# Output weight remainders on VectorE, three of them inside the experts' last step, and one input weight remainder on GpSimd

## What is computed

```
attn = softmax(q k^T / 8 - slope * distance, masked) v        # 2 x 8 heads, 768 tokens, 64 wide
x    = sum_e p[:, e] * (relu(attn @ w1[e]) @ w2[e])           # 1536 tokens, 512 -> 1024 -> 512, 4 experts
h    = x @ w_in                                               # 512 -> 1024
solu = h * softmax(h)
ln   = (solu - mean(solu)) / sqrt(var(solu) + 1e-6) * g_ln
out  = ln @ w_out                                             # 1024 -> 512
```

## Time and profile before

| | |
|---|---|
| time, median of 3 runs | 753.35 us |
| the profiled execution | 753.5 us, span 751.7 us |
| TensorE busy | 744.6 us, 99% of the span, 3994 passes |
| TensorE's weight loads busy | 652.9 us, 87% |
| VectorE busy | 525.5 us, 70% |
| ScalarE busy | 218.9 us, 29% |
| GpSimd busy | 341.0 us, 45% |
| granted TensorE clock | 1.000 |

### The profile page before, as it was taken

One profiled execution on the slowest core, in us unless ns is written; L12 is line 12 of the kernel. 1 busy time (PEld: TensorE's weight loads), 2 busy tenths in 40 slices (PEclk: granted clock), 3 DMA queues, 4 the chain that ended last, 5 costly groups with the idle time before them and its releaser, 6 DMA issues. The chain is left out here.

```text
span 751.7 us, 12616 instructions
## 1 busy us (share of the span) xinstructions
PE 744.6 (99%) x3994; PEld 652.9 (87%) x3994; DVE 525.5 (70%) x1042; ACT 218.9 (29%) x414; POOL 341.0 (45%) x326
## 2 busy tenths in 40 slices
PE   9999999999999999999999999999999999999998
PEld 8888899899898998989988898898898877888876
DVE  5677767676666766767666676676767799867772
ACT  5677641111111111111211112111113743433332
POOL 4367546253542535425354253543535974442400
PEclk9999999999999999999999999999999999999999
DMA  9756310100101000010000100000022100000001
GB/s 263 194 142 167 105 31 2 56 29 29 31 26 56 28 28 28 28 56 28 28 28 28 56 28 28 28 28 0 1 112 66 49 0 15 15 29 28 16 28 42
DMA packets 39106, 37.15 MB, mean 49 GB/s; under 512 B 14497, under 2 KB 31905, under 8 KB 39073
## 3 DMA queue, kind: packets, MB, share of 16 engines
q1 hardware_dynamic: 37472, 34.64, 15.0%
q10 hardware_dynamic: 1600, 2.10, 0.8%
HBM read 33.59 MB, written 3.15 MB: 49 GB/s over the span
## 5 line engine op out<-in xcount | busy, mean ns | idle before, releaser
L809 PE MATMUL y_ps<-w2s,hs 128*128 128x512 f32 x1140 | 286.0, 395 | 0.1
L789 PE MATMUL p_ps<-xs,ws 128*128 128x384 f32 x1344 | 255.2, 336 | 0.0
L809 PEld LDWEIGHTS y_ps<-w2s,hs 128*128 128x128 f32 x1140 | 212.4, 188 | 41.0 <-DVE acc L1474 0.6
L789 PEld LDWEIGHTS p_ps<-xs,ws 128*128 128x128 f32 x1344 | 237.6, 188 | 11.0
L1474 DVE SCALAR_TENSOR_TENSOR acc<-y_ps,pr,acc 128x512 f32<-128x512 f32 x178 | 133.0, 748 | 79.6 <-PE y_ps L809 78.6
L1121 ACT ACTIVATE hs<-hs_sum 128x384 fp32r<-128x384 f32 x128 | 67.4, 527 | 353.6 <-DVE hs_sum L1442 238.9
L1461 DVE SCALAR_TENSOR_TENSOR hs<-hs_sum,hs 128x384 fp32r<-128x384 f32 x128 | 93.2, 737 | 4.3 <-ACT hs L1121 2.2
L577 POOL TENSOR_TENSOR ws_sum<-raw_sum 128x256 f32<-128x256 f32 x16 | 11.8, 739 | 146.8 <-PE p_ps L789 146.0
L608 POOL CAST w2s<-raw_sum 128x1024 fp32r<-128x1024 f32 x16 | 16.9, 1056 | 86.1 <-PE y_ps L809 86.1
L1134 ACT ACTIVATE neg_s<-neg_s,row 128x256 f32<-128x256 f32 (+1 forms) x96 | 42.2, 483 | 26.0 <-DVE row L1493 25.9
L1493 DVE CUSTOM_DVE_ANT_0 neg_s<-s_ps,bias 128x256 f32<-128x256 f32 (+1 forms) x96 | 34.3, 399 | 20.2 <-PE s_ps L823 18.1
(11 more groups left out here) (152 smaller groups left out, 971.2 us busy)
## 6 DMA issues: line engine op xcount, KB each, us to landing
raw_sum<-in_w SPq DMA_DIRECT2D x28, 512.0 KB, 3.5
qk<-in_qkW SPq DMA_DIRECT2D x24, 256.0 KB, 3.7
qk<-in_qkW SPq DMA_DIRECT2D x24, 128.0 KB, 4.1
v_sb<-in_v SPq DMA_DIRECT2D x16, 192.0 KB, 3.0
out<-o_sb SPq DMA_DIRECT2D x12, 256.0 KB, 2.0
raw_sum<-in_w ACTq DMA_DIRECT2D x4, 512.0 KB, 7.0
raw_sum<-in_w_in SPq DMA_DIRECT2D x1, 2048.0 KB, 8.0
wout_lo_a_sum<-in_w_out SPq DMA_DIRECT2D x1, 1792.0 KB, 7.6
```

Source lines behind the costliest of these rows:

```text
L789: mm = nc.tensor.matmul(bank, ws[slot][:, w, part, kk, :], xs[:, 2 * bt + kk, x, part, :], start=(kk == 0 and w == 1 and x == 1), stop=(kk ...
L809: mm = nc.tensor.matmul(mixed_at(s, t), hs[bt][:, h, b, tok], w2s[slot][:, w, f, :], start=(f == 0 and h == 1 and w == 1), stop=(f == 1 an ...
```

## The change

ScalarE's scaling in place (L1264) is gone, and all eight chunks of `w_out` are scaled and rounded in one instruction. The remainders of all eight are made on VectorE by the operation that chunks 4 to 7 had. Those of chunks 0, 1 and 2 stand inside VectorE's list for step 31, those of 3 and 4 between the last four `add_up`, those of 5 to 7 where they were. The sixth input weight remainder goes from VectorE to GpSimd. VectorE's loop over the steps ends one round (four steps) earlier, and steps 28 to 31 are written out.

```diff
-    WIN_POOL = 5
+    WIN_POOL = 6
...
-            def split_wout(c):
-                pool.wait_ge(wouthi_ready, c + 1)
-                pool.sem_inc(pool_waited, 1)
-                nc.gpsimd.tensor_tensor(wout_lo(c), wout_raw(c), f32(wout_hi(c)), ALU.subtract).then_inc(wout_ready, 1)
...
             for q in range(2):
-                for c in range(2):
-                    split_wout(2 * q + c)
                 x2_sums(q)
                 x2_los(q)
...
                         if s == 0:
-                            pe.wait_ge(wout_ready, FC // 2)
-                            pe.wait_ge(wout_split, FC // 2)
+                            pe.wait_ge(wout_ready, FC)
...
             def wout_hi_part(c):
-                if c < FC // 2:
-                    act.wait_ge(wout_scaled, c + 1)
-                    nc.scalar.activation(wout_hi(c), wout_raw(c), ACT.Copy).then_inc(wouthi_ready, 1)
-                else:
-                    nc.scalar.activation(wout_hi(c), wout_raw(c), ACT.Copy, scale=gain_sb[:, c:c + 1]
-                                         ).then_inc(wouthi_ready, 1)
+                nc.scalar.activation(wout_hi(c), wout_raw(c), ACT.Copy, scale=gain_sb[:, c:c + 1]).then_inc(wouthi_ready, 1)
...
             for c in range(FC // 2):
-                scale_wout(c)
+                wout_hi_part(c)
             relu_hi(LAST, 3, 1)
-            for c in range(FC // 2):
-                wout_hi_part(c)
             relu_hi(LAST, 2, 1)
...
+            def wout_lo_part(c):
+
+                if c == 0:
+                    dve.wait_ge(gain_loaded, 16)
+                dve.wait_ge(wouthi_ready, c + 1)
+                nc.vector.scalar_tensor_tensor(wout_lo(c), wout_raw(c), gain_sb[:, c:c + 1], f32(wout_hi(c)),
+                                               ALU.mult, ALU.subtract).then_inc(wout_ready, 1)
+
             def halve(a, i):
...
                 third_sum(s, i)
+                if isinstance(a, int) and s == LAST:
+                    wout_lo_part(0)
                 add_up(s - 1, 3, 1 - bt, expert, first)
...
                 lower_block(s, i)
+                if isinstance(a, int) and s == LAST:
+                    wout_lo_part(1)
+                    wout_lo_part(2)
                 right_block(s, i)
...
-            with dve.Fori(1, STEPS // 4) as a:
+            with dve.Fori(1, STEPS // 4 - 1) as a:
                 for i in range(4):
                     halve(a, i)
+            for i in range(4):
+                halve(STEPS // 4 - 1, i)
...
             for t in range(4):
                 add_up(LAST, t, 1, E - 1)
-                if t in (0, 2):
-                    win_lo_part(WIN_POOL + t // 2)
+                if t == 1:
+                    win_lo_part(WIN_POOL)
+                    wout_lo_part(3)
+                if t == 3:
+                    wout_lo_part(4)
...
             def first_pair():
-                wout_lo_part(4)
                 wout_lo_part(5)
```

More of the change, by code:

```diff
@@ L360, in attention_experts_solu_kernel @@
         winlo_dve = sem("winlo_dve")
-        wout_scaled = sem("wout_scaled")
         wouthi_ready = sem("wouthi_ready")
         wout_ready = sem("wout_ready")
-        wout_split = sem("wout_split")
         p_done = sem("p_done")
@@ L1255, in wout_hi_part @@
             def wout_hi_part(c):
-                if c < FC // 2:
-                    act.wait_ge(wout_scaled, c + 1)
-                    nc.scalar.activation(wout_hi(c), wout_raw(c), ACT.Copy).then_inc(wouthi_ready, 1)
-                else:
-                    nc.scalar.activation(wout_hi(c), wout_raw(c), ACT.Copy, scale=gain_sb[:, c:c + 1]
-                                         ).then_inc(wouthi_ready, 1)
-            def scale_wout(c):
-                nc.scalar.activation(wout_raw(c), wout_raw(c), ACT.Copy, scale=gain_sb[:, c:c + 1]).then_inc(wout_scaled, 1)
+                nc.scalar.activation(wout_hi(c), wout_raw(c), ACT.Copy, scale=gain_sb[:, c:c + 1]).then_inc(wouthi_ready, 1)
             act.wait_ge(win_loaded, 16)
@@ L1662, in _, with win_lo_part @@
                 attend_wide()
+            def win_lo_part(at):
+                n = WIN_ORDER[at]
+                dve.wait_ge(winhi_ready, at + 1)
+                nc.vector.tensor_tensor(win_lo_at(n), win_sum_at(n), f32(win_hi[:, n]), ALU.subtract
+                                        ).then_inc(winlo_dve, 1)
+            def wout_lo_part(c):
[4 more added lines that the diff above has]
+                                               ALU.mult, ALU.subtract).then_inc(wout_ready, 1)
             def halve(a, i):
@@ L1688, in _ @@
                 halve(0, i)
-            with dve.Fori(1, STEPS // 4) as a:
+            with dve.Fori(1, STEPS // 4 - 1) as a:
                 for i in range(4):
                     halve(a, i)
-            def win_lo_part(at):
-                n = WIN_ORDER[at]
-                dve.wait_ge(winhi_ready, at + 1)
-                nc.vector.tensor_tensor(win_lo_at(n), win_sum_at(n), f32(win_hi[:, n]), ALU.subtract
-                                        ).then_inc(winlo_dve, 1)
-            def wout_lo_part(c):
-                if c == FC // 2:
-                    dve.wait_ge(gain_loaded, 16)
-                dve.wait_ge(wouthi_ready, c + 1)
-                nc.vector.scalar_tensor_tensor(wout_lo(c), wout_raw(c), gain_sb[:, c:c + 1], f32(wout_hi(c)),
-                                               ALU.mult, ALU.subtract).then_inc(wout_split, 1)
+            for i in range(4):
+                halve(STEPS // 4 - 1, i)
             for t in range(4):
                 add_up(LAST, t, 1, E - 1)
-                if t in (0, 2):
-                    win_lo_part(WIN_POOL + t // 2)
+                if t == 1:
[3 more added lines that the diff above has]
+                    wout_lo_part(4)
             def negated(q, n, m, half, other):
```

## The result

The changed kernel took 754.58 us at the median of 20 executions (753.84 to 755.53), the kernel before 753.41 (753.29 to 753.88, 20 executions). The ratio is 1.0015, interval 1.0009 to 1.0022: 1.2 us slower, a difference clear of zero but inside the 1.5 us that the prediction counts as no change. The forecast was 754.0, its range 752.5 to 755.6.

What follows compares the result with a forecast made beforehand. TensorE, 99% busy, was taken as the bound, with VectorE's chain second and setting the end after 616. TensorE's net +0.6 and VectorE's +0.8 gave some +0.7 us on 753.35: 754.05, stated as 754.0, range 752.5 to 755.6.

Steps and rivals of the forecast that it cites:

- Output remainder 0: VectorE, step 31: held by GpSimd's second input remainder, runs 589.3 to 590.0; `lower_block` 0.5 us late, nothing waits.
- Output remainders 1 and 2: VectorE ahead of `right_block`, step 31: GpSimd blocks them, `mix(31, 0)` starts about 598.0, TensorE loses 2.85 us.
- The rule of turns: Two-SBUF-input VectorE and SBUF-reading GpSimd instructions exclude each other; whoever began finishes, then the waiter goes; up to 2.5 us each.
- What comes back: TensorE up to the second pair's first `up`: waits of 0.19, 0.1, 0.3 and 1.67 us (for L742) vanish.
- the sum there: TensorE at the second pair's first `up`: 2.85 us lost less the returned waits leaves +0.6 us.
- VectorE's chain in the second pair: Tail: `largest(0)` waits out the second L742, `solu_part(0)` starts +0.8 us later, and that shift moves the end.
- At nothing: ScalarE's dropped roundings, the moved input remainder, remainders 3 and 4, steps written out: 0, code fetch bounds -0.2 and +1.
- Rival A: Step 31: blocking weaker than scheduled, `mix(31, 0)` only 0.1 us late, -2.2 us, 751.2; chance 0.09.
- Rival B: Ahead of `mix(31, 0)`: GpSimd gets two more turns of 0.74, TensorE loses 4.3, total +2.2, 755.6; chance 0.15.
- Rival C, the clock: New 2.85 us gap before `mix(31, 0)`: clock falls to 1.2 GHz, two slow `mix` add +2.8, 756.9; chance 0.05.

Runs made afterwards that it cites:

- e3_pool5: The changed kernel with the sixth input weight remainder back on VectorE, so GpSimd has five instead of six; 753.87 us, ratio 1.0005.
- e4_behind_relu: The changed kernel with output remainders 1 and 2 moved behind both `relu_lo` of step 31; 753.28 us, ratio 0.9996.
- e8: The repeated run: the changed kernel once more, without an edit; 754.39 us, ratio 1.0013 against the kernel before.
- e1_filled_gap: The changed kernel with nine unread matmuls in TensorE's gap ahead of `mix(31, 0)`; 754.01 us, ratio 1.0006.
- e5_pool_splits_late: The kernel before, with two of GpSimd's four output splits moved behind `spread(0)`, past the second `L742`; 753.45 us, ratio 1.0001.
- e9_pool_splits_gated: e6 with GpSimd's two splits held back until VectorE has done three small two-operand instructions (L1779 to L1781); 752.01 us, ratio 0.9983 against the kernel before.
- e10_mid_filled: e6 with six unread matmuls ahead of `up(1, 5)`, where TensorE waited 1.86 us; 753.12 us, ratio 0.9994 against the kernel before.
- e2_written_out: The kernel before, with only VectorE's last four steps written out instead of looped; 753.67 us, ratio 1.0002.
- e6: The kernel before, with two of GpSimd's four output splits moved directly behind the second pair's `L742`; 753.46 us, ratio 0.9998.
- e7: The changed kernel with output remainder 3 also ahead of `right_block` in step 31; 756.33 us, ratio 1.0038 against the kernel before.

## Why the prediction was right, and where it was not

The forecast schedule held nearly row by row, and at full clock it gave the number: 754.1 against 754.05 worked out on the median. Two parts of that are luck. The growth of the distance in the trace is 0.52, and 0.7 was forecast; the rest lies in when `mix(30, 5)` starts, which differs between executions (593.61 to 594.22 in the traces) and for which the prediction has no term. And the median stayed inside "no change" only because fewer than half of the executions had a fall of the clock: those that did are 2.0 us above the kernel before.

- *Output remainder 0.* Forecast to end at 590.0 behind GpSimd's second input remainder; it ended at 589.86 after 2.40 us. Right.
- *Output remainders 1 and 2.* Forecast to issue at 593.1 and end at 596.95; they issued at 592.97 and ended at 596.53. `mix(31, 0)` at 597.64 (forecast 598.0), a loss of 2.6 us for the 2.85 forecast. The rule of turns was right, and the turns came somewhat sooner than written: the sixth input remainder ended at 594.86 (595.0), the sum between the two remainders at 595.99 (596.3). `e3_pool5` showed that 1.8 of the loss came with the sixth input remainder, which the step names, and `e4_behind_relu` that it is the place ahead of `right_block` that exposes TensorE to it.
- *What comes back.* The wait for `L742` went. At full clock 2.53 us came back up to `up(1, 1)` (distance 20.56 before, 20.62 in the repeated run), where 2.26 were forecast: 0.27 at `up(0, 1)`, 0.08 at the next turn, 0.45 in the first pair, 1.76 at `L742`, against 0.02 more in `mix`. So the sum there was +0.06 and not +0.6. That term was mis-sized, by 0.26 in the loss and 0.27 in the return. Most of the second comes from a misread base: 0.44 us from `turn_x` to the next pass, taken as undisturbed, is not. A later pair of the same trace has 0.35, and the pairs of the changed kernel have 0.35 or 0.36:

```profile
617.15 0.60 PE L950 MATMUL xr_ps<-ident,acc 128*128 128x128 f32 x4
617.50 0.48 PE L1028 MATMUL up_ps<-win_hi,x 128*128 128x512 f32 x1
```

- *VectorE's chain in the second pair.* It saved the number, since it and not TensorE's list sets the end. `largest(0)` issued at 613.81 and was held to 615.79 (forecast 614.0 and 615.9); `solu_part(0)` came 0.54 to 0.67 later, forecast 0.8; the distance to the end grew by 0.52. The 0.5 us that TensorE had regained went into its next wait for `stats`, 0.74 in place of 0.25. The traces without a fall of the clock show which chain sets the end. Change of distance against the kernel before, us:

| | `up(1, 1)` | `solu_part(0)` | `up(1, 5)` | end |
|---|---|---|---|---|
| changed (`e8`) | +0.06 | +0.54 | +0.55 | +0.52 |
| `e1_filled_gap` | +0.09 | +0.57 | +0.59 | +0.63 |
| `e3_pool5` | +0.48 | +0.37 | +0.39 | +0.37 |
| `e4_behind_relu` | -0.67 | -0.19 | -0.16 | -0.15 |
| `e5_pool_splits_late` | -2.14 | -1.53 | -1.51 | +0.04 |
| `e9_pool_splits_gated` | -2.18 | -1.57 | -1.55 | -1.48 |
| `e10_mid_filled` | -2.15 | -1.54 | -0.47 | -0.46 |

The end does not follow `up(1, 1)`. It follows `solu_part(0)`, but for `e10`, where that instruction itself is held up for 1.1 us by the splits, and `e5`, where VectorE's chain is held up behind it.

- *At nothing.* The steps written out cost nothing that shows (`e2_written_out`).
- *Rival A* fell with the first remainder's 2.40 us. *Rival B* did not occur, no further turn was lost. Its price was added up wrongly: 2.85 and two turns of 0.74 make 4.33, less the return of 2.26 some +2.1, which is 755.4 and not 755.6; the upper end of the range hangs on it.
- *Rival C, the clock.* This is what the prediction had wrong. It got a chance of 0.05, because nothing in the trace showed a fall. It happened in 8 of 20 executions and in 3 of 11 of the repeated run. Its price was also mis-sized: not two `mix` at half speed (+2.8), but 3.4 us of them, 1.52 us at TensorE and 1.35 at the end (755.45 to 754.1). The first four passes ran at full clock before the fall. With this share the median of 20 comes to 754.58 rather than 754.1. `e1_filled_gap` and `e10_mid_filled` point to TensorE's idleness as the cause: the same delays with TensorE busy, and no fall in 22 executions, with the chips as the one rival left.

The Trainium skill's warning ("TensorE: Matmul & The Clock Gate", section "Why this matters for your kernels") that a gap can bring the lower clock back was cited in the prediction as something no run showed. Here the runs show it, at idle times of 2.4 and 1.9 us. The row of that section is about longer gaps than these, so here the measurement decides.

What stays open: why only a part of the executions fall. TensorE's longest idle time near the place was 1.5 us in the kernel before (none of the 80 executions with a clock on record below 0.999), 1.9 in `e6` (7 of 11), 2.4 in the changed kernel (11 of 31), 3.6 in `e7` (4 of 5). With so few executions neither an even growth with the idle time nor its absence is shown. No run moved one gap in time alone, and no filled kernel is on record beside its unfilled one on the same chip.

## What to carry to other kernels

Price a VectorE instruction with two SBUF operands by what GpSimd does in that moment, and schedule both engines as taking turns: remainders of one form were 0.74 or 2.40 us. Work taken off an engine that TensorE waits for gives back only as much as the other engine in the chain allows, so look one wait further before counting it; here 2.5 us came back and 0.5 us of them were lost again. A gap of some 2 us in TensorE's list carries the risk of the lower clock, 1.35 us more here in a third of the executions; if it cannot be closed, it can be filled.

## What was unexpected of the hardware

- The exclusion of GpSimd and VectorE holds for instructions of one column too: 1.21 us for one of 0.16 (`e5`), 1.98 for `largest` (0.16 without GpSimd), while `BATCH_NORM_STATS2` over 512 columns with one operand kept its 0.69 beside GpSimd (`e9`). In these rows it is the operands, not the size, that count.
- The order in time of the same two GpSimd instructions was worth 1.4 us (`e9` to `e5`, 752.01 to 753.45), more than the 1.2 that the whole change cost.
- The fall of the clock has no fixed place against the gap: 0.8 us after work had resumed in the changed kernel (598.5, first pass 597.64), 0.25 after in `e6`, and 0.6 before it, inside the gap, in `e7`. It lasted 3.4 us in all three, so it costs TensorE's passes behind the gap in each case, though not equally: 24 passes of `mix` took 7.22 us in the changed kernel, 6.98 in `e7` and 5.70 at full clock.
